# A second expert layer in tiles of 512 token rows instead of 256

## What is computed

```
attn   = max(z @ z.T / S, 0) ** 2            # 4 batches of S = 2496
x      = u * (attn @ v)                      # 9984 x 256
layer 1: tokens with x @ w_skip > 0 go to expert argmax(x @ w_gate); x += gate * (relu(x @ w1[e]) @ w2[e])
layer 2: every token goes to expert e = argmax(x @ w_gate2 + bias[modality])
         out = gate * (relu(x @ w1[e]) @ w2[e])          # w1: 256 x 1024, w2: 1024 x 256
```

## Time and profile before

| | us |
|---|---|
| median of 3 runs | 1544.33 (1540.39 to 1544.65) |
| the profiled execution | 1541.97 |
| its span in the profile | 1540.3 |

### The profile page before, as it was taken

The page is one execution under the profiler, slowest core; times in us unless marked ns, Lnnn a source line. Parts: engine busy times, 40 slices in busy tenths (PEclk is TensorE's granted clock), DMA queues, the critical chain, the costliest instruction groups (busy, mean ns, idle before and its releaser), DMA issues.

```text
span 1540.3 us, 37994 instructions
## 1 busy us (share of the span) xinstructions
PE 1504.4 (98%) x13409; PEld 1373.3 (89%) x13409; DVE 1000.2 (65%) x2414; ACT 757.4 (49%) x1463; POOL 397.2 (26%) x370
## 2 busy tenths in 40 slices
PE   8999999999999999999899999999999999999995
PEld 7778887788877887878799999999999999999995
DVE  7988977889778988877666666663333333333332
ACT  6676766667666767665344444443222222222221
POOL 4133321334223324212222222224211111111111
PEclk9999999999999999999999999999999999999998
DMA  5302030112202020201533343323111111111110
GB/s 117 97 30 63 28 97 29 62 35 63 83 29 64 28 84 27 84 30 31 173 113 135 134 162 132 105 97 98 49 49 42 42 56 47 42 42 49 48 42 27
DMA packets 60107, 106.40 MB, mean 69 GB/s; under 512 B 18183, under 2 KB 32018, under 8 KB 59980
## 3 DMA queue, kind: packets, MB, share of 16 engines
q1 hardware_dynamic: 41788, 46.66, 11.0%
q0 software_dynamic: 18192, 58.13, 10.9%
HBM read 75.35 MB, written 30.94 MB: 69 GB/s over the span
## 4 chain that ended last, share of the span: by engine, by line
PE 90%; DMA 3%; issue 2%; POOL 1%; DVE 1%; ACT 1%; SPq 1%; POOLq 0%; DVEq 0%; ACTq 0%
PE pO L1248 31%; PE pS L1459 23%; PE pO L1442 23%; PE pS L1237 9%; PE pT L1388 2%; DMA raw<-in_v_dram 2%; PE pT L1296 1%; PE pO L1257 1%; PE pM L1306 1%; PE pO L1370 0%; DMA raw<-in_z_dram 0%; POOL VL L504 0%; DMA out_dram<-xrow,tok_at 0%; DMA A<-in_w2t_dram 0%; POOL VL L466 0%
## 5 line engine op out<-in xcount | busy, mean ns | idle before, releaser
L786 ACT ACTIVATE AH<-pO 128x512 fp32r<-128x512 f32 x252 | 144.1, 598 | 460.4 <-PE pO L1442 460.4
L1442 PE MATMUL pO<-ZH,VH 128*128 x2016 | 351.1, 286 | 1.4 <-DVE VL L1157 0.7
L1459 PE MATMUL pS<-VL,AH 128*128 128x256 f32 (+1 forms) x2016 | 323.9, 283 | 1.6 <-DVE AL L1163 1.6
L958 DVE TENSOR_TENSOR AL<-A,AH 128x512 fp32r<-128x512 f32 (+1 forms) x400 | 305.0, 762 | 13.7
L1248 PE MATMUL pO<-AH,VH 64*128 64x512 f32 (+1 forms) x1520 | 301.1, 387 | 3.7 <-DVE xT L867 2.3
L1248 PE MATMUL pO<-AH,VL 64*128 64x512 f32 (+1 forms) x1520 | 298.6, 383 | 0.0
L1248 PE MATMUL pO<-AL,VH 64*128 64x512 f32 (+1 forms) x1520 | 298.0, 382 | 0.0
L1163 DVE SCALAR_TENSOR_TENSOR AL<-pO,AH 128x512 fp32r<-128x512 f32 x252 | 170.0, 689 | 187.0 <-ACT AH L786 186.9
L1442 PEld LDWEIGHTS pO<-ZH,VH 128*128 128x128 f32 x2016 | 286.4, 192 | 3.2 <-issue 3.2
L660 ACT ACTIVATE R<-pS 128x512 f32<-128x512 f32 (+1 forms) x400 | 213.1, 586 | 146.8 <-PE pS L1237 146.3
L1459 PEld LDWEIGHTS pS<-VL,AH 128*128 128x128 f32 x2016 | 275.7, 189 | 1.8 <-DVE AL L1163 1.8
(11 more groups left out here) (196 smaller groups left out, 1523.1 us busy)
## 6 DMA issues: line engine op xcount, KB each, us to landing
raw<-in_w_dram POOLq DMA_DIRECT2D x22, 1024.0 KB, 7.8
xin<-token_rows SPq DMA_DIRECT2D x65, 268.0 KB, 2.7
uT<-in_u_dram SPq DMA_DIRECT2D x16, 512.0 KB, 3.7
A<-in_w2t_dram POOLq DMA_DIRECT2D x8, 1024.0 KB, 5.9
raw<-in_v_dram SPq DMA_DIRECT2D x4, 1152.0 KB, 5.8
raw<-in_v_dram SPq DMA_DIRECT2D x4, 768.0 KB, 7.8
raw<-in_z_dram SPq DMA_DIRECT2D x8, 368.0 KB
token_rows<-pad_row SPq DMA_DIRECT2D x10, 268.0 KB
```

The lines of the kernel that those rows point to most:

```text
L786: s_.activation(hH[p], pO[:, p * 512:(p + 1) * 512], ACT.Relu).then_inc(q.h_hi, 1)
L958: v_.tensor_tensor(AL[k % NBUF][:, 0:n], A[k % NA][:, 0:n], AH[k % NBUF][:, 0:n].bitcast(F32), ALU.subtract).then_inc(al_ready, 1)
L1442: last = t_.matmul(pO[:, bank * 512 + fi * TT:bank * 512 + (fi + 1) * TT], w[h][:, kd, f * P:(f + 1) * P], x[:, ds(par, 1), kd, :].rearran ...
L1459: last = t_.matmul(pS[s][:, 0:width], a[p][:, fi * TT + s * P:fi * TT + (s + 1) * P], w[h][:, f, 0:width], start=(f == 0 and n == 0), stop ...
```

## The change

The first layer keeps its code (`for ph in range(1)`). The second layer gets code of its own, `second_phase`, on ScalarE, VectorE and TensorE, with tiles of 512 rows:

- layer 1 moves 512 columns in each pass, and its 8 sums go round a ring of three banks (pS[0], pS[1], pM); the six passes of a sum follow one another in one bank;
- layer 2 has w2's high and low part side by side as one moving operand of 512 columns for the high part of h (results in one bank of pO for each of four sub-tiles: high product in the first 256 columns, low product in the last 256), and a pass of 256 columns for the low part of h, added to the first half;
- ScalarE scales the second half by the gate into xrow (`low_part`), VectorE adds the first half times the gate; each sub-tile is scattered by itself;
- the transposes of the next tile come in two halves of four, each followed by its cast and its split, since pT is one bank;
- of the rows only gate and token number are kept (`marks`); the rows are loaded into `xin2`, in the place of the transposed w2 of the first layer, so SyncE waits until that has been used.

```diff
+TT2 = 512
+TILE = (TT, TT2)
+RING = 3
+        XTH2 = ZH[:, 0:2 * KD * TT2].rearrange("p (b k t) -> p b k t", b=2, k=KD)
+        w2hl = [VL[:, s * VW:s * VW + 2 * WD * YW].rearrange("p (m f d) -> p m f d", m=2, d=YW) for s in range(2)]
+        hring = [pS[0], pS[1], pM]
+        xin2 = A_all[:, 0:SUB2 * ROW].rearrange("p (s d) -> p s d", s=SUB2)
...
+                    if ph == 1:
+                        sp.wait_ge(gcols_made, E)
...
-                                wait(q.y2_out, t + 1)
-                                for s_ in range(SUB):
-                                    g_.indirect_dma_start(out, bass.IndirectOffsetOnAxis(tok_at[:, s_:s_ + 1], 0), x2a[:, s_, 0:D], None,
+                                for s_ in range(SUB2):
+                                    wait(q.y2_out, SUB2 * t + s_ + 1)
+                                    g_.indirect_dma_start(out, bass.IndirectOffsetOnAxis(tok_at2[:, s_:s_ + 1], 0), xrow[:, s_, 0:D], None,
...
+                def take_half(t, par, kd):
+                    act.wait_ge(q.x_transposed if kd else q.x_half, t + 1 + kd)
+                    s_.copy(XTH2[:, ds(par, 1), kd, :].rearrange("p o t -> p (o t)"), pT[:, :]).then_inc(q.xt_hi, 1)
...
+                def low_part(t, par, s):
+                    act.wait_ge(q.y_made, SUB2 * t + s + 1)
...
+                    s_.activation(xrow[:, s, 0:D], pO[:, s * QW + D:(s + 1) * QW], ACT.Copy,
+                                  scale=marks[:, ds(par, 1), s, 0:1].rearrange("p o m -> p (o m)")).then_inc(q.y_low, 1)
...
+                            h_high(0)
+                            h_high(1)
+                            h_high(2)
+                            h_high(3)
+                            take_half(t + 1, (t + 1) % 2, 0)
+                            h_high(4)
+                            h_high(5)
+                            take_half(t + 1, (t + 1) % 2, 1)
+                            keep_marks(t + 1, (t + 1) % 2)
+                            h_high(6)
+                            h_high(7)
+                            with act.If(t == lo):
+                                with act.If(hi < total):
+                                    for n in range(WP):
+                                        split_high(turn_ + 1, 1 - h, n)
+                            for s in range(SUB2):
+                                low_part(t, t % 2, s)
...
+                            for s in range(SUB2):
+                                dve.wait_ge(q.y_low, SUB2 * t + s + 1)
+                                v_.scalar_tensor_tensor(out=xrow[:, s, 0:D], in0=pO[:, s * QW:s * QW + D], scalar=marks[:, ds(par, 1), s, 0:1].rearrange("p o m -> p (o m)"),
+                                                        in1=xrow[:, s, 0:D], op0=ALU.mult, op1=ALU.add).then_inc(q.y2_out, 1)
+                            dve.wait_ge(q.y2_out, SUB2 * t + SUB2)
+                            dve.sem_inc(q.y_out, 1)
...
+                def transpose_half(t, kd):
+                    pe.wait_ge(q.x_loaded, 16 * t + 16)
+                    if not (isinstance(t, int) and t == 0 and kd == 0):
+                        pe.wait_ge(q.xt_split, 2 * t + kd)
...
+                transpose_half(0, 0)
+                transpose_half(0, 1)
+                keep_warm(pS[0], 48)
...
+                            def layer1(f):
+                                pe.wait_ge(q.h_split, NF * t + (NF - 2 + f if f > 1 else NF - 1 + f))
+                                n = 0
+                                for kd in range(KD):
+                                    for w, x in ((w1h, XTH2), (w1h, XTL2), (w1l, XTH2)):
+                                        last = t_.matmul(hring[f % RING][:, :], w[h][:, kd, f * P:(f + 1) * P],
+                                                         x[:, ds(par, 1), kd, :].rearrange("p o t -> p (o t)"), start=(n == 0), stop=(n == 3 * KD - 1))
...
+                            def layer2(f):
+                                pe.wait_ge(q.h_split, NF * t + NF + f + 1)
+                                if f == 0:
+                                    pe.wait_ge(q.y_out, t + 1)
+                                for s in range(SUB2):
+                                    rows = slice(s * P, (s + 1) * P)
+                                    t_.matmul(pO[:, s * QW:(s + 1) * QW].rearrange("p (m d) -> p m d", m=2), AH[f][:, rows], w2hl[h][:, :, f, 0:D],
+                                              start=(f == 0), stop=(f == NF - 1), skip_group_check=True)
+                                    last = t_.matmul(pO[:, s * QW:s * QW + D], AL[f][:, rows], w2h[h][:, f, 0:D],
+                                                     start=False, stop=(f == NF - 1), skip_group_check=True)
...
```

More of the change, by code:

```diff
@@ L43 @@
 SUB = TT // P
-CAP = N + TT
+TT2 = 512
+SUB2 = TT2 // P
+TILE = (TT, TT2)
+NF = F // P
+RING = 3
+CAP = N + TT2
 SPARE = 3 * P
@@ L360, in load_x @@
                         sp.wait_ge(q.x_kept, t + 1)
-                        sp.dma_start(xin[:, :, :], xs[ds(row, TT), :].rearrange("(p s) d -> p s d", s=SUB)).then_inc(q.x_loaded, 16)
+                        sp.dma_start(xin2 if ph else xin[:, :, :], xs[ds(row, rows_in), :].rearrange("(p s) d -> p s d", p=P)).then_inc(q.x_loaded, 16)
                     sp.wait_ge(early_ready, ph + 1)
@@ L402, in _ @@
                                 with sp.Fori(first, hi) as t:
-                                    load_x(t, within(e * CAP + (t - lo) * TT, 0, GR * CAP - TT))
+                                    load_x(t, within(e * CAP + (t - lo) * rows_in, 0, GR * CAP - rows_in))
                             with sp.If(hi == total):
-                                load_x(total, within(e * CAP, 0, GR * CAP - TT))
+                                load_x(total, within(e * CAP, 0, GR * CAP - rows_in))
                         lo = hi
@@ L727, in _ @@
             exp_chunk(CHUNKS)
-            for ph in range(2):
+            for ph in range(1):
                 q = PH[ph]
@@ L815, in _ @@
+            total0 = total
+            second_phase()
         @block.vector
@@ L1012, in plan_counts @@
             def plan_counts():
-                f(v_.tensor_scalar(here[:, :], cnt[:, E:GR], float(TT), None, ALU.is_ge))
+                f(v_.tensor_scalar(here[:, :], cnt[:, E:GR], float(TT2), None, ALU.is_ge))
                 f(v_.tensor_tensor(pair[:, :, :], less[:, :, :], here[:, None, :].to_broadcast([P, E + 1, E]), ALU.mult))
@@ L1180, in _ @@
                             dve.wait_ge(q.h_used, 4 * t + 8)
-                            if ph == 0:
-                                dve.wait_ge(q.staged, t + 1)
-                            else:
-                                dve.wait_ge(q.stored, STORED + 32 * t)
+                            dve.wait_ge(q.staged, t + 1)
                             dve.wait_ge(q.x_kept, t + 2)
@@ L1209, in _, with second_phase, low_half, h_low @@
                     finish_groups(1)
+            def second_phase():
+                q = PH[1]
+                dve.sem_inc(q.h_split, NF)
+                dve.sem_inc(q.y_out, 1)
+                dve.wait_ge(cum_ready, 2)
+                def low_half(t, par, kd):
+                    dve.wait_ge(q.xt_hi, 2 * t + kd + 1)
+                    v_.tensor_tensor(XTL2[:, ds(par, 1), kd, :].rearrange("p o t -> p (o t)"), pT[:, :],
+                                     XTH2[:, ds(par, 1), kd, :].rearrange("p o t -> p (o t)").bitcast(F32), ALU.subtract).then_inc(q.xt_split, 1)
+                for kd in range(KD):
+                    low_half(0, 0, kd)
+                lo = 0
+                for at in range(E):
+                    hi = end_of(dve, 1, at)
+                    with dve.If(lo < hi):
+                        with dve.Fori(lo, hi) as t:
+                            def h_low(f):
+                                dve.wait_ge(q.h_hi, NF * t + f + 1)
+                                v_.scalar_tensor_tensor(out=AL[f][:, :], in0=hring[f % RING][:, :], scalar=0.0,
+                                                        in1=AH[f][:, :].bitcast(F32), op0=ALU.max, op1=ALU.subtract).then_inc(q.h_split, 1)
+                            for f in range(4):
+                                h_low(f)
+                            low_half(t + 1, (t + 1) % 2, 0)
+                            h_low(4)
+                            h_low(5)
+                            low_half(t + 1, (t + 1) % 2, 1)
+                            h_low(6)
+                            h_low(7)
+                            par = t % 2
+                            dve.wait_ge(q.stored, STORED + 16 * SUB2 * t)
+                            dve.wait_ge(q.x_kept, t + 2)
+                            v_.tensor_copy(tok_at2[:, :], marks[:, ds(par, 1), :, 1:2].rearrange("p o s m -> p (o s m)"))
+                            for s in range(SUB2):
[3 more added lines that the diff above has]
+                            dve.wait_ge(q.y2_out, SUB2 * t + SUB2)
+                            dve.sem_inc(q.y_out, 1)
```

(8 more changed lines are left out.)

126 lines of the change are left out of this document (99 added, 27 removed).

## The result

The changed kernel takes 1531.9 us (median of 5 runs, 1529.94 to 1534.54), the kernel before in runs beside them 1543.81 us (1539.53 to 1544.65): a ratio of 0.9931, 95% interval 0.9917 to 0.9945. Forecast were 1530.0 us and "faster". The time came out within 2 us, but by luck in good part: the sum behind it is not right, as the two profiles show when they are cut at the same four places.

| us | ahead | start | stretch | tail | span |
|---|---|---|---|---|---|
| before | 1043.60 | 5.19 | 475.92 | 15.64 | 1540.3 |
| changed | 1039.09 | 10.58 | 461.50 | 18.98 | 1530.1 |
| difference | -4.5 | +5.4 | -14.4 | +3.3 | -10.2 |
| forecast | 0 | +4.2 | -20.2 | +1.7 | -14.3 |

What follows compares the result with a forecast made beforehand. TensorE's own passes were taken to bound the second expert layer. Stretch -20.2, start +4.2 and tail +1.7 sum to -14.3 us, from 1544.3 to 1530.0 us; own range 1522 to 1540, with hidden loads 1511 to 1540.

Steps and rivals of the forecast that it cites:

- ahead: Part up to the first expert layer's last prefix step on TensorE; instructions kept, forecast 0.
- start: From that prefix step to the second layer's first layer 1 matmul; transposes in halves and slow warming, +4.2 us.
- stretch: From the second layer's first layer 1 matmul to TensorE's last matmul; fewer, wider passes, 455.7 against 475.9, -20.2 us.
- tail: From TensorE's last matmul to the span's end; four scatters one by one instead of two, +1.7 us.
- the extra: Time of a TensorE pass beyond its columns; 11 to 16 ns at widths 256 to 512, taken as paid per pass.
- the attention's pairs: Attention's side-by-side 64-row matmuls of 512 columns, 226.5 ns a pair; taken as price of the new 512-column passes.
- The two runs: Layer 2's 512-column operand as two separate runs of 256; second run taken at 0, range 0 to 12 ns each.
- the slow rival: Two-run operand of layer 2's wide passes is read more slowly; decides from 22 ns a pass; chance 0.10.
- Hidden loads: Rival: the extra is weight loading, hidden by 512-column passes at 216.0 ns; 1513.2 us; chance 0.22.
- The edge: Between tiles, layer 2 waits for VectorE's last read of pO; no cost, 2.5 us to spare; rival 1540 us, 0.08.
- the switch of experts: First tile, low-part scaling queued on ScalarE behind four weight copies; still inside the 4.08 us cover, 0.3 us charged.
- "0" for the rest: The first expert layer and the attention keep their instructions, so no change in time was forecast there.

Runs made afterwards that it cites:

- widths run: Changed kernel plus groups of sixteen fp32r passes of several widths, banks and operands after the last tile; 512 columns with 128 weight columns: 226.9 to 233.8 ns a pass.
- after_again: The changed kernel run once more, unedited; 1530.95 us, ratio 0.9931 to the kernel before.
- warm_leave: Changed kernel with 64 matmuls on ones between the first transposes' halves, 16 behind, and GpSimd leaving empty turns in one branch; 1528.08 us, ratio 0.9914.
- before_again: The kernel before run once more, unedited, for a second profile; 1538.59 us.
- before_cap: Kernel before with token_rows as large as the changed kernel's, 512 rows more than the tokens instead of 256; 1541.33 us, ratio 0.9996.
- warm_first: Changed kernel with 64 matmuls on ones between the first transposes' halves and 16 behind, instead of 48 behind; 1529.42 us, ratio 0.9926.
- first_two_banks: warm_leave with the second half of the first tile's transposes in bank pS[1] and 72 matmuls on ones after both halves; 1523.81 us, ratio 0.989.
- before_scatter_first: Kernel before, second layer: GpSimd sends an expert's first tile's scatters ahead of the next expert's weight split; 1538.26 us, ratio 0.9974.

## Why the prediction was right, and where its steps were not

The time was missed by 1.9 us, but the layer's own terms add up to -5.7 instead of -14.3 us in the pair of profiles, and what filled the gap was not in the sum. The direction and the mechanism were right; that the time came so close is luck.

- **The stretch** (-20.2 forecast, -14.4 measured). The mechanism holds: TensorE alone bounds it, the extra is paid per pass, fewer passes gain. The term that was mis-sized is the price of a 512-column pass, 226.5 ns from the attention's pairs. Layer 1's cost 229 and layer 2's wide ones 231.6 ns, 0.12 + 0.16 = 0.28 us a tile, 5.6 us in 20. The attention's price lies at the low end of what the widths run gives for 512 columns (226.9 to 233.8). The sentence that this price already has the single bank in it is not borne out: one bank costs 229.4 ns there, two by turns 226.9. That it explains layer 1 is argued, since the layer wasn't run with two banks.
- **The two runs**: taken at 0, bounded by 12 ns; 6.9 at most were seen, and joining them gained nothing. The 22 ns from which the slow rival decides are far off. The Trainium skill ("PSUM — Partial Sum Buffer", Specifications (TRN2)) says that any non-contiguous access pattern slows matmuls significantly, in its row on PSUM's cachelines; these passes have an unbroken output and two runs in SBUF, and show 3 per cent.
- **Hidden loads**: refuted by the widths run, where 512 columns cost 226.9 to 233.8 ns and weights of half the columns make them no cheaper. The support that the prediction saw in the earlier trace rows was a misreading: at half clock 128 and 192 columns cost the same 213.3 ns. By the Trainium skill ("TensorE: Matmul & The Clock Gate", Back-to-back issue gap) an isolated matmul of 512 columns would cost 213.3 + 2.5 = about 216 ns at full clock, an estimate; 226.9 to 233.8 were measured here for fp32r passes in a row, and the measurement decides.
- **The edge**: right, 2.4 us to spare against 2.5, no wait in any tile. The tile with the switch of experts took 23.23 us, 0.18 more; 0.3 had been charged.
- **The start** (+4.2 forecast, +5.4 and +4.6 measured): right in each step and inside its bounds (2.6 to 6.2); the clock was at 0.50 for 6.83 us, so all 48 matmuls on ones ran slow. The start before isn't fixed either: 5.2 us in two profiles of the old layer, 6.3 and 6.5 in the two in which the clock fell. And the idle time isn't all that the fall goes by: in after_again it came 0.2 us into the 3.72 us, in the changed kernel's first profile 2.8 us into the 3.73.
- **The tail** (+1.7 forecast, +3.3 measured): the scatters were right to 0.1 us; the step that failed is that what follows them was taken as unchanged. From the last scatter to its DRAIN GpSimd needs 1.7 us more, and warm_leave shows that this time is its walk through the empty turns.
- **"0" for the rest**: the part ahead scatters by 5.8 us between executions, about as much as the layer gains. And the earlier trace rows showed the old stall at its shortest; its 1.6 us were counted, its 2.8 us in the median not. By medians the kernel gains 11 to 12 us. In the profiles the layer (start, stretch and tail) wins 5.7 to 6.9 us over before and before_again, and 9.9 to 11.0 over before_cap, whose old layer had the longest stall and two falls of the clock. So a part of the remainder is such longer cases of the old layer, another fits the shift of the part ahead; so few profiles don't show the shares, nor that the shift is more than chance.

## What to carry to other kernels

Where TensorE is busy in every moment, cut the number of passes, and price the new pass from the nearest shape with the same bank pattern, weights and neighbours: 2.5 to 5 ns a pass were 5.6 us here. Price the ends of a stage as well as its middle: a longer first tile, a clock that falls while it is prepared and a longer way out of the program took back 8.7 of 14.4 us, and two lines at the start returned some 3 of these in the profile. Before a gain is put down to a change, profile the kernel before twice: the part that nobody touched moved by as much as the layer gained.

## What the runs showed that was not expected

- In fp32r with 128 columns of weights a pass cost 12.7 to 20.4 ns over its columns at every width from 256 to 512 in the widths run, in uneven steps (448 columns: 19.6; 384: 13.8). At the half clock 128, 192 and 256 columns cost the same, 213.3 ns.
- The granted clock fell to 0.50 for 6.8 us around a start with 3.73 us of idle time, and it stayed at 1.00 there in warm_first and warm_leave, with matmuls on ones in that gap; but in first_two_banks, before_cap and before_scatter_first it fell, for 3.4 us, with only 1.6 us of idle time ahead.
- GpSimd's final DRAIN took 6.8 to 6.9 us in every kernel, and the way to it from the last scatter 0.3 to 0.4 us where it left the empty turns in one branch, 3.8 to 5.8 us in the kernel before and the changed one.
